# Low-rank mixing over tokens: last products of a batch set together, three PSUM banks for them in the third batch, and the fifth token tile of U's products over all 128 partitions

## What is computed

```python
phi(x) = concat(exp(p), exp(-p))            # p = x @ w_phi, less the row maximum of |p|; 8 heads of 64
attn   = phi(q) (phi(k)^T v) / (phi(q) . sum phi(k) + 1e-6)
h      = relu(attn @ w_in)                  # 512 -> 1024
x      = (h * sigmoid(conv3(h))) @ w_out    # 1024 -> 512
u      = x + ((x^T @ U) @ V)^T              # the mixing over tokens: U is 576 x 32, V is 32 x 576
out    = u + relu(u @ w_ch1) @ w_ch2        # 512 -> 2048 -> 512
```

## Time and profile before

| what | value |
|---|---|
| runs, median (lowest to highest) | 902.22 us (899.07 to 903.17) |
| the profiled execution, its own time | 901.18 us |
| its span in the trace | 899.6 us |
| mean granted clock of TensorE | 0.995 |
| busy PE / DVE / ACT / POOL | 98% / 42% / 33% / 11% |
| PE's waits that the trace lists (each name's total) | 0.2 to 2.5 us |

### The profile page before, as it was taken

How to read it: one execution, slowest core, us unless ns; L and a number is a source line. 1 busy time by engine, 2 the same in 40 slices (tenths; PEclk the granted TensorE clock), 3 DMA queues, 4 the chain that set the end, 5 groups by cost and what they waited for, 6 DMA issues and landing times.

```text
span 899.6 us, 14982 instructions
## 1 busy us (share of the span) xinstructions
PE 884.7 (98%) x6242; PEld 874.0 (97%) x6242; DVE 374.0 (42%) x641; ACT 292.5 (33%) x581; POOL 101.2 (11%) x67
## 2 busy tenths in 40 slices
PE   8999999999999999999999999999999999999997
PEld 7899999999999999999999999999999999999997
DVE  5565574365763467733794442122122122122111
ACT  3545454345642355423542331111211111111111
POOL 5541121000210002100240001010010010010000
PEclk8999999999999999999999999999999999999999
DMA  7999612327322093042572621201201201201001
GB/s 184 271 265 244 188 55 76 84 72 252 102 80 81 21 292 94 1 165 91 191 240 100 197 72 36 71 1 36 71 1 36 71 1 36 71 1 36 36 1 35
DMA packets 106033, 88.96 MB, mean 99 GB/s; under 512 B 61040, under 2 KB 92656, under 8 KB 103920
## 3 DMA queue, kind: packets, MB, share of 16 engines
q1 hardware_dynamic: 105216, 87.82, 32.8%
q10 hardware_dynamic: 752, 0.20, 0.1%
HBM read 70.18 MB, written 17.83 MB: 98 GB/s over the span
## 4 chain that ended last, share of the span: by engine, by line
PE 88%; DVE 7%; issue 3%; ACT 2%; POOL 0%; ACTq 0%; DVEq 0%
PE kvb L1110 8%; PE qnb L1053 7%; PE qnb L1054 7%; PE qnb L1055 7%; PE qnb L1140 7%; PE pjb L1053 6%; PE pjb L1055 5%; PE pjb L1054 5%; PE mb L1053 5%; PE mb L1055 5%; PE mb L1054 5%; PE tpb L1053 2%; PE kvb L1055 2%; PE tpb L1054 2%; PE kvb L1053 2%
## 5 line engine op out<-in xcount | busy, mean ns | idle before, releaser
L974 DVE SCALAR_TENSOR_TENSOR c_lo<-qnb,c_hi 128x384 fp32r<-128x384 f32 x94 | 52.4, 558 | 282.6 <-ACT c_hi L751 282.6
L751 ACT ACTIVATE c_hi<-qnb 128x384 fp32r<-128x384 f32 x94 | 46.3, 492 | 294.2 <-PE qnb L1055 290.3
L1053 PE MATMUL qnb<-u_hi,w_b 128*128 128x384 f32 x384 | 129.8, 338 | 0.0
L1055 PE MATMUL qnb<-u_hi,w_b 128*128 128x384 f32 x384 | 128.4, 334 | 0.0
L1054 PE MATMUL qnb<-u_lo,w_b 128*128 128x384 f32 x384 | 128.4, 334 | 0.0
L520 POOL TENSOR_TENSOR g_lo<-cv,g_hi 128x576 fp32r<-128x576 f32 x31 | 46.2, 1491 | 344.8 <-DVE g_hi L793 344.8
L1053 PEld LDWEIGHTS qnb<-u_hi,w_b 128*128 128x128 f32 x384 | 72.1, 188 | 0.1
L1054 PEld LDWEIGHTS qnb<-u_lo,w_b 128*128 128x128 f32 x384 | 72.2, 188 | 0.0
L1055 PEld LDWEIGHTS qnb<-u_hi,w_b 128*128 128x128 f32 x384 | 72.1, 188 | 0.0
L808 DVE TENSOR_REDUCE nm<-pjb 128x4 f32<-128x512 f32 (+1 forms) x80 | 50.6, 632 | 46.7 <-PE pjb L1055 46.4
L1053 PE MATMUL mb<-x_hi,winr 128*128 128x288 f32 x224 | 69.3, 309 | 0.0
(11 more groups left out here) (254 smaller groups left out, 1916.5 us busy)
## 6 DMA issues: line engine op xcount, KB each, us to landing
winr<-wi_dram SPq DMA_DIRECT2D x32, 512.0 KB, 4.2
woutr<-wo_dram SPq DMA_DIRECT2D x15, 1024.0 KB, 5.3
stage<-in_moe_w_ch_dram SPq DMA_DIRECT2D x32, 256.0 KB, 4.0
us<-u_dram SPq DMA_DIRECT2D x6, 768.0 KB, 4.8
ua<-u_dram SPq DMA_DIRECT2D x6, 768.0 KB, 4.7
qr<-in_q_dram SPq DMA_DIRECT2D x32, 128.0 KB, 2.7
vt<-in_v_dram SPq DMA_DIRECT2D x32, 128.0 KB, 3.2
wi_dram<-aw SPq DMA_DIRECT2D x8, 512.0 KB, 5.6
```

Source lines behind the costliest of these rows:

```text
L751: nc.scalar.activation(c_hi[:, j % CR, :], CH[j % 2][:, 0:TW], ACT.Relu).then_inc(s_chh, 1)
L974: nc.vector.scalar_tensor_tensor(out=c_lo[:, j % CR, :], in0=CH[j % 2][:, 0:TW], scalar=0.0, in1=c_hi[:, j % CR, :].bitcast(F32), op0=ALU. ...
L1053: mm(o, a_hi, b_hi, start=start, stop=False)
L1055: return mm(o, a_lo, b_hi, start=False, stop=stop)
```

## The change

1. `tu`, `x1_high` and `x1_low` no longer slice the fifth token tile: all five tiles use 128 partitions. Rows 0 to 63 of `u_st` are zero there, so the sum is the same. `x1_rows` goes.
2. In the first two batches w = 2 of group 1 moves from (19, 0) to (19, 2), where w = 3 stands already.
3. In the third batch w = 0, 1 and 2 of group 0 are done together at (15, 0), behind that piece's outputs, in banks M1, PJ0 and PJ1; w = 3 moves from (16, 1) to (16, 0), in M1. Before w = 1 stands a wait for the last use of PJ by attention (s_dif at its final count), before w = 3 one for the addition of w = 0.
4. In the straight-line part the wait for these additions moves from the second half of the hidden layer's first step to ahead of `x1_by_token`, which now follows in PJ.

```diff
-    HU_AT = {(14, 2): (0, 0), (15, 0): (0, 1), (15, 2): (0, 2), (16, 1): (0, 3),
-             (18, 1): (1, 0), (18, 2): (1, 1), (19, 0): (1, 2), (19, 2): (1, 3)}
+    HU_AT = {(14, 2): (0, (0,)), (15, 0): (0, (1,)), (15, 2): (0, (2,)), (16, 1): (0, (3,)),
+             (18, 1): (1, (0,)), (18, 2): (1, (1,)), (19, 2): (1, (2, 3))}
+
+    HU_LAST = {(15, 0): (0, (0, 1, 2)), (16, 0): (0, (3,))}
+
+    def hu_at(b, m, piece):
+        return (HU_LAST if b == B - 2 else HU_AT).get((m, piece), (None, ()))
...
-    def hu_bank(g, w):
-        return 1 if g == 0 else w % 2
-
...
-    def x1_rows(i):
-        return token_tile(2 * i)[1] if i == XP - 1 else slice(0, P)
...
+        def hu_bank(b, g, w):
+            if b == B - 2 and w in (1, 2):
+                return PJ[:, w - 1, :]
+            return M[:, 1 if g == 0 else w % 2, :]
...
             def x1_high(b, g, i, bank):
-                rows, ts = x1_rows(i), x1_tiles(i)
+                ts = x1_tiles(i)
                 act.wait_ge(s_xm, XP * (2 * b + g) + i + 1)
                 act.wait_ge(s_tu, 2 * b + g)
-                copy(xt_hi[rows, ts.start:ts.stop, :],
-                     bank[rows, 0:len(ts) * GC].rearrange("p (t c) -> p t c", c=GC)).then_inc(s_xmh, 1)
+                copy(xt_hi[:, ts.start:ts.stop, :],
+                     bank[:, 0:len(ts) * GC].rearrange("p (t c) -> p t c", c=GC)).then_inc(s_xmh, 1)
...
-                if (m, piece) in HU_AT:
-                    g, w = HU_AT[m, piece]
-                    add_hu(b, g, w, M[:, hu_bank(g, w), :])
+                g, ws = hu_at(b, m, piece)
+                for w in ws:
+                    add_hu(b, g, w, hu_bank(b, g, w))
...
                 for t in range(UT):
-                    rows = token_tile(t)[1]
-                    st = u_st[rows, t, :, :].rearrange("p a r -> p (a r)")
-                    mm(bank[:, 0:GC], st, xt_hi[rows, t, :], start=(t == 0), stop=False)
-                    last = mm(bank[:, 0:GC], st, xt_lo[rows, t, :], start=False, stop=(t == UT - 1))
+                    st = u_st[:, t, :, :].rearrange("p a r -> p (a r)")
+                    mm(bank[:, 0:GC], st, xt_hi[:, t, :], start=(t == 0), stop=False)
+                    last = mm(bank[:, 0:GC], st, xt_lo[:, t, :], start=False, stop=(t == UT - 1))
...
-                if (m, piece) in HU_AT:
-                    g, w = HU_AT[m, piece]
-                    if g == 0 and w or w > 1:
+                g, ws = hu_at(b, m, piece)
+                for w in ws:
+                    if b == B - 2 and w == 1:
+                        pe.wait_ge(s_dif, PERIOD * NP)
+                    elif b == B - 2 and w == 3:
+                        pe.wait_ge(s_u, 2 * CC * b + 1)
+                    elif b < B - 2 and (g == 0 and w or w > 1):
                         pe.wait_ge(s_u, 2 * CC * b + (w if g == 0 else CC + w - 1))
-                    hu(b, g, w, M[:, hu_bank(g, w), :])
+                    hu(b, g, w, hu_bank(b, g, w))
...
             transposes("o", NP - 1)
+            pe.wait_ge(s_u, 2 * CC * (b - 1) + CC)
             for i in range(XP):
                 x1_by_token(b - 1, 1, i, XLB[i])
             for j in range(J1):
                 for half in range(2):
-                    if j == 0 and half:
-                        pe.wait_ge(s_u, 2 * CC * (b - 1) + CC)
-                    elif j > 1:
+                    if j > 1:
                         pe.wait_ge(s_rel, 2 * (J1 * b + j - 2) + half + 1)
```

More of the change, by code:

```diff
@@ L879, in x1_low @@
             def x1_low(b, g, i, bank):
-                rows, ts = x1_rows(i), x1_tiles(i)
+                ts = x1_tiles(i)
                 dve.wait_ge(s_xmh, XP * (2 * b + g) + i + 1)
-                sub(xt_lo[rows, ts.start:ts.stop, :],
-                    bank[rows, 0:len(ts) * GC].rearrange("p (t c) -> p t c", c=GC),
-                    xt_hi[rows, ts.start:ts.stop, :].bitcast(F32)).then_inc(s_xml, 1)
+                sub(xt_lo[:, ts.start:ts.stop, :],
+                    bank[:, 0:len(ts) * GC].rearrange("p (t c) -> p t c", c=GC),
+                    xt_hi[:, ts.start:ts.stop, :].bitcast(F32)).then_inc(s_xml, 1)
             def mix_low(b, g, bank):
```

## The result

The changed kernel takes 897.02 us (median of 11 runs, 894.87 to 899.09), the kernel before 901.26 us beside it (median of 11, 899.07 to 903.17). The ratio is 0.9953, 95% interval 0.9939 to 0.9967: a small gain, but the interval leaves no gain out. The forecast was 898.0 us and the ratio 0.9953.

What follows compares the result with a forecast made beforehand. PE, busy for 98% of the span, was taken as the bound, so its stalls are time lost. Terms 2.61 + 1.33 + 0.32 = 4.26 us from 902.22 gave 898.0 us, ratio 0.9953, range 895.8 to 899.9.

Steps and rivals of the forecast that it cites:

- The fifth tile, 2.61 us: U's products in all four batches: at 128 rows the fifth tile's long steps shrink to 0.12 us, saving 2.61 us.
- The limits by `mix` in the first two batches: Group 1, first two batches: w = 0 waits for `mix`, so each gains 0.19 us of the 0.38.
- a drain at each change of form and at each product of the narrow form: U's fifth tile: 64-row products keep the load from running ahead, giving steps of 0.21 to 0.22 us, not 0.12.
- The bound with one more DVE copy: Copies for U's fifth tile: without work to cover them, one more DVE copy of 0.43 us for each group.
- Third batch, 1.33 us: Last transpose to query contraction, w = 0, 1, 2 together: 4.48 us falls to 3.15, saving 1.33.
- The margin of the query features: Third batch: ACT ends the query features about 413.2, PE reaches the contraction at 414.0, leaving 0.8 us.
- First two batches, 0.16 us each: w = 2 moved behind the transposes: query transposes then wait for `dq` on DVE, saving 0.16 us a batch.
- The sum, 4.26 us: Whole kernel: 2.61 for the fifth tile, 1.33 for the third batch and 0.32 for the first two.
- The narrow form is the cause: U's fifth tile; the rival denied it: steps stay at 0.21 us, only 1.65 us gained, 900.6 us; chance 0.06.
- no wait took the place of the removed ones: V's products, first three batches; the rival expected new waits, V's part shrinking to 0.5 us, 899.1 us; chance 0.15.
- PE waits for no load in the fourth batch: Fourth batch's hidden layer; the rival expected late `winr` loads and a slower 904.3 to 907.5 us; chance 0.03.
- That more would be gained: Whole kernel; rival: slower first steps go and the `mix` chain moves further, 5.2 us gained, 896 to 897; chance 0.12.

Runs made afterwards that it cites:

- low64: Changed kernel with the fifth tile's products over partitions 0 to 63 instead of all 128; the four stretches take 0.60, 0.60, 0.78 and 0.70 us more.
- tile_only: Kernel before with only the fifth token tile widened to all 128 partitions; the four stretches together gain 2.43 us.
- narrow6: Changed kernel with the fifth tile's two products done three times over partitions 64 to 127; stretches 118.23, 118.23, 73.55 and 430.95 us.
- third_only: Kernel before with only the third batch's w = 0, 1, 2 together in three banks and the moved wait; third stretch loses 1.25 us.
- low_later: Changed kernel with group 1's mix_low moved behind the next tick's softmax maxima on DVE in the first two batches; those stretches lose 0.48 and 0.61 us.
- banks_only: Changed kernel with the third batch's V products at their four old places but in the new banks; third stretch takes 0.71 us more.
- shared: Changed kernel with the third batch's w = 0, 1, 2 all in bank M1, each waiting for the addition before it; third stretch takes 1.68 us more.
- w2_only: Kernel before with only group 1's w = 2 moved behind the transposes in the first two batches; those stretches lose 0.15 and 0.14 us.
- rows96: Changed kernel with the fifth tile's products over partitions 0 to 95; stretches 116.73, 116.74, 71.84 and 429.18 us.
- combined: Changed kernel with mix_low later on DVE and group 1's w = 0 moved to w = 1 in the first two batches; 896.01 us, ratio 0.9924.

## Why the prediction was right, point by point

- **The fifth tile, 2.61 us.** Right in sum: 2.68 against low64. (Without it the sum is 4.26 - 2.61 = 1.65 us; the 1.64 of the prediction is a slip.) The limits by `mix` in the first two batches came out (0.57 to 0.59 in tile_only, 0.57 forecast). The mechanism "a drain at each change of form and at each product of the narrow form" was wrong in its second half: narrow6 shows products inside the narrow form at full pace. With two of them per group both readings give the same time, so the sum could not tell. In the third batch `mix` limits the gain too as long as w = 0 stands at its old place, which I overlooked for tile_only (0.14 us short); in the whole change it doesn't count. The bound with one more DVE copy was not needed, as low64 shows.
- **Third batch, 1.33 us.** The path from the last transpose to the contraction takes 3.16 us, the sum said 3.15. The margin of the query features held: 0.90 us, forecast 0.8. Alone (third_only) the same path takes 3.18 us, 1.30 less than before, and the stretch gains 1.25; the 0.05 between them stays unexplained.
- **First two batches, 0.16 us each.** 0.15 and 0.14 alone. That DVE becomes the bound there was right, and low_later shows it: DVE's order alone gives another 0.5 us.
- **The sum, 4.26 us.** 4.27 in the stretches. The terms are right to under 0.1 us each; that they add up to within 0.01 is luck, since the first two stretches gave 0.04 and 0.02 more and the last one 0.04 less. The median's distance, 901.26 - 897.02 = 4.24 us, agrees, but so closely only by luck: each kernel's own runs spread over some 4 us, and the interval of the ratio allows 3.0 to 5.5 us. The time itself came out 0.98 us under the forecast 898.0 because the forecast started from the median of three runs, 902.22, and that of eleven is 901.26.
- **The rivals.** The narrow form is the cause; no wait took the place of the removed ones beyond the one at `dq`; PE waits for no load in the fourth batch of the changed kernel. That more would be gained (5.2 us, 896 to 897 us) fell by the stretches, 4.27 us; by the median of the runs alone, 897.02 us, it could not have been told from the forecast.
- The last stage kept all that was gained ahead of it, as assumed.

## What to carry to other kernels

A partial last tile can be cheaper at full height with zeros than at half: two products of 64 rows among products of 128 cost 0.39 us more, though they do less work, and this shows only in steps from start to start, not in the list of waits. A wait that is booked at 0.55 us can cost 0.82, since a part of it lies in the printed length of the product ahead and the step behind it is longer too; and grouping products that share a bank only lines the waits up, unless each gets a bank of its own. When a change is worth tenths of a microsecond, cut the traces at landmarks: here they repeat within about 0.1 us where whole runs differ by 4.

## What the runs showed beyond what was expected

Most of the spread between these traces comes from some 20 us at their start. The granted clock from 10 to 20 us, on average, and the time of the first landmark:

| version (one trace each) | clock, 10 to 20 us | first landmark |
|---|---|---|
| after, banks_only, low_later | 1.00 | 158.81, 158.88, 158.93 |
| shared, third_only | 1.00 | 159.48, 159.55 |
| before, tile_only, w2_only | 0.66 | 160.84, 160.87, 160.86 |
| rows96, narrow6 | 0.59 | 162.21, 162.24 |
| low64, combined | 0.56 or 0.55 | 162.73, 162.76 |

All these versions are the same up to that point. PE had been granted 2.4 GHz in the first 10 us of each and was busy for 5.9 to 7.2 us of them; before and after alike, it began at 1.8 us and stood idle for 1.87 us just ahead of 10.6 us, waiting for ACT. The clock then fell to 1.2 GHz for a part of the next 10 us in seven of the twelve traces, and in the four of the last two lines the mean from 20 to 40 us is still 0.95 to 0.97. From 40 us on it is 1.00 up to the landmark in all twelve. What decides it is open: busy time in those first 10 us doesn't order them (7.08 us in low64, which fell, 6.59 in after, which didn't), and no run was made for it.

From the first line of the table to the last it is up to 3.95 us, nearly as much as the whole change. The mean clocks of the eleven runs of the changed kernel, of which only the fastest has a trace, fit this: the five at 0.998 and above took 894.87 to 896.70 us, the six at 0.995 and below 897.02 to 899.09.

Not all of it is the clock. The second line of the table is 0.6 to 0.7 us behind the first at the same clock, and in its two traces PE waits for a load of `winr` in the first batch, near 84 us, for 0.6 us in shared and 0.3 in third_only; the three traces of the first line have no such wait. So a load of `winr` can come late, though the trace of the kernel before shows no wait for one; the change has no part in it, since the code there is the same.
